# Scores of the dense stage's RWKV units on 64 by 64 quarters of TensorE, without the masked quarter

## The reference

```python
# r, k, v: 4 x 8 x 768 x 48 (batch, heads, tokens, head width); w, u: 8 x 48
for t in range(S):
    cur = einsum('bhd,bhe->bhde', u * k[t], v[t])
    y[:, :, t] = einsum('bhd,bhde->bhe', r[t], state + cur)
    state = w * state + einsum('bhd,bhe->bhde', k[t], v[t])
x = y as 3072 x 384
x = (silu(x @ w_gate) * (x @ w_val)) @ w_out           # dense, 384 -> 1536 -> 384
out = gate * sigmoid * (relu(x @ w1[e]) @ w2[e])        # e: the expert of the row's largest logit
```

## Time and profile before

| what | value |
|---|---|
| median of 3 runs | 874.12 us (874.0 to 876.14) |
| the profiled execution, its own time | 870.95 us |
| its span, first to last instruction | 869.0 us |
| TensorE busy | 844.3 us, 97% |
| VectorE busy | 537.6 us, 62% |
| ScalarE busy | 314.9 us, 36% |
| GpSimd busy | 175.3 us, 20% |
| granted TensorE clock, mean | 0.992 |

### The profile page before, as it was taken

How to read it: one execution, slowest core, us unless ns; L and a number is a source line. 1 busy time by engine, 2 the same in 40 slices (tenths; PEclk the granted TensorE clock), 3 DMA queues, 4 the chain that set the end, 5 groups by cost and what they waited for, 6 DMA issues and landing times. The chain is left out here.

```text
span 869.0 us, 16447 instructions
## 1 busy us (share of the span) xinstructions
PE 844.3 (97%) x6107; PEld 739.0 (85%) x6107; DVE 537.6 (62%) x1063; ACT 314.9 (36%) x500; POOL 175.3 (20%) x141
## 2 busy tenths in 40 slices
PE   7699999999999999999999999999999999999995
PEld 6578888788878888878788878899899999999995
DVE  8667746564566445544444446469969777887770
ACT  1223223111311131112211221347457666687651
POOL 3543302242133403240101001003121101111010
PEclk9799999999999999999999999999999999999999
DMA  9764420352024302340011002537986668766700
GB/s 362 269 210 135 149 92 12 88 172 66 0 65 137 131 1 66 103 133 1 10 46 38 1 2 63 230 137 255 376 325 246 238 245 321 261 247 249 274 17 19
DMA packets 37282, 125.78 MB, mean 145 GB/s; under 512 B 4236, under 2 KB 21056, under 8 KB 31600
## 3 DMA queue, kind: packets, MB, share of 16 engines
q1 hardware_dynamic: 32848, 108.14, 35.3%
q0 software_dynamic: 3520, 9.87, 3.0%
q10 hardware_dynamic: 864, 7.08, 2.2%
HBM read 107.26 MB, written 18.88 MB: 145 GB/s over the span
## 5 line engine op out<-in xcount | busy, mean ns | idle before, releaser
L1607 PE MATMUL bank<-X1H,WH 128*128 128x512 f32 x432 | 169.1, 392 | 2.0 <-DVE YS L1008 1.7
L1607 PE MATMUL bank<-X1L,WH 128*128 128x512 f32 x432 | 168.2, 389 | 0.0
L1607 PE MATMUL bank<-X1H,WL 128*128 128x512 f32 x432 | 168.2, 389 | 0.0
L1243 DVE TENSOR_TENSOR TT<-bank,SG 128x512 f32<-128x512 f32 x72 | 49.7, 691 | 137.5 <-ACT SG L807 137.4
L807 ACT ACTIVATE SG<-bank 128x512 f32<-128x512 f32 x72 | 43.0, 598 | 240.0 <-PE bank L1607 240.0
L737 ACT ACTIVATE AH<-PP 128x512 fp32r<-128x512 f32 (+1 forms) x78 | 46.1, 598 | 158.4 <-DVE PP L1248 158.4
L1607 PEld LDWEIGHTS bank<-X1H,WH 128*128 128x128 f32 x432 | 81.1, 188 | 20.5 <-issue 3.4
L1607 PEld LDWEIGHTS bank<-X1H,WL 128*128 128x128 f32 x432 | 81.1, 188 | 17.1
L1607 PEld LDWEIGHTS bank<-X1L,WH 128*128 128x128 f32 x432 | 81.1, 188 | 16.5
L1653 PE MATMUL bank<-AH,WH 128*128 128x512 f32 (+1 forms) x234 | 91.5, 391 | 0.0
L1655 PE MATMUL bank<-AH,WL 128*128 128x512 f32 (+1 forms) x234 | 87.8, 375 | 0.0
(11 more groups left out here) (229 smaller groups left out, 1798.5 us busy)
## 6 DMA issues: line engine op xcount, KB each, us to landing
W_EVEN<-w SPq DMA_DIRECT2D x20, 1536.0 KB, 8.3
W_ODD<-w SPq DMA_DIRECT2D x18, 1536.0 KB, 8.1
RK_IN<-unit_rk SPq DMA_DIRECT2D x18, 736.0 KB, 5.7
V_IN<-unit_v SPq DMA_DIRECT2D x18, 448.0 KB, 3.4
STG<-w_dense ACTq DMA_DIRECT2D x6, 1152.0 KB, 6.5
mixed<-YS SPq DMA_DIRECT2D x40, 96.0 KB, 2.1
X<-mixed SPq DMA_DIRECT2D x5, 768.0 KB, 4.5
XG_ODD<-store SPq DMA_DIRECT2D x9, 394.0 KB, 8.2
```

What stands on the lines that cost most here:

```text
L1243: tt(TT[:, :], GATE_PS[:, :], SG[:, :], ALU.mult).then_inc(gate_free, 1)
L1607: last = mm(bank_[:, :], lhs[:, f, m, k * P:k * P + P], rhs[:, k, :], start=(x == 0), stop=(x == len(terms) - 1))
```

## The change

Two functions change, for the 18 units of the dense stage alone. In `scores` each head's matmul is cut by keys: the first 64 keys (`EARLIER`) against all 128 queries, the last 64 keys (`LATER`) against the last 64 queries. The quarter of late keys and early queries, which the mask makes zero, is no longer computed. Both pieces have 64 weight columns, so each lies on one quarter of the array. In `mask_scores` the product of each bank is cut in the same way, into 64x512 and 64x4x64; the late-key, early-query part of AM is not written by these units. It holds the zeros that the units ahead of the stage wrote there. A `nop` now carries the wait for `y_added`.

```diff
+EARLIER, LATER = slice(0, P // 2), slice(P // 2, P)
...
                 for half in range(2):
                     dve.wait_ge(scores_ready, 2 * u.i + half + 1)
-                    tt(u.am[:, half, :, :], u.scores[half][:, :].rearrange("p (j t) -> p j t", j=PAIRS),
-                       mask.unsqueeze(1).broadcast_to([P, PAIRS, P]), ALU.mult).then_inc(masked, 1)
+                    made = u.scores[half][:, :].rearrange("p (j t) -> p j t", j=PAIRS)
+                    strict = mask.unsqueeze(1).broadcast_to([P, PAIRS, P])
+                    if u.start:
+                        last = tt(u.am[:, half, :, :], made, strict, ALU.mult)
+                    else:
+                        tt(u.am[EARLIER, half, :, :], made[EARLIER, :, :], strict[EARLIER, :, :], ALU.mult)
+                        last = tt(u.am[LATER, half, :, LATER], made[LATER, :, LATER], strict[LATER, :, LATER], ALU.mult)
+                    last.then_inc(masked, 1)
...
                     pe.wait_ge(y_added, u.behind)
+                    pe.nop(nofuse=True)
                 for s in range(PAIRS):
                     for x in range(2):
                         a = Head(HEAD_AT[x][s])
-                        last = mm(u.scores[x][:, a.keys], u.kw[a.rows, a.keys], u.rw[a.rows, a.keys], start=True, stop=True)
+                        r, w = u.rw[a.rows, a.keys], u.kw[a.rows, a.keys]
+                        if u.start:
+                            last = mm(u.scores[x][:, a.keys], w, r, start=True, stop=True)
+                        else:
+                            to = u.scores[x][:, a.keys]
+                            mm(to[EARLIER, :], w[:, EARLIER], r, start=True, stop=True)
+                            last = mm(to[LATER, LATER], w[:, LATER], r[:, LATER], start=True, stop=True)
                         if s == PAIRS - 1:
                             last.then_inc(scores_ready, 1)
```

## The result

| | before | after |
|---|---|---|
| median of 6 runs each, same chip | 874.06 us (872.27 to 876.14) | 868.95 us (867.91 to 870.28) |
| the profiled execution, its own time | 870.95 us | 867.91 us |
| its span | 869.0 us | 866.1 us |
| TensorE busy | 844.3 us | 839.8 us |
| VectorE busy | 537.6 us | 559.6 us |

The ratio is 0.994, with an interval of 0.9924 to 0.9957: faster by more than the 0.3% that can be told. So the change is worth some 3 us, as the two spans say (2.9), and the first comparison was the luckiest of three.

What follows compares the result with a forecast made beforehand. TensorE's own instruction list was taken as the bound; 17 units x 0.21 us = 3.6 us saved, VectorE's added work hidden, so the median goes from 874.1 to 870.5 us, range 869.0 to 874.8.

Steps and rivals of the forecast that it cites:

- The border goes: TensorE between key sums and scores: sharing quarters removes both losses at the shape change, 0.21 us a unit with 0.02 streaming gain.
- 17 units x 0.21 = 3.6 us.: TensorE, dense stage: 17 of the 18 changed units each save 0.21 us, 3.6 us in all.
- The range, 874.0 - 4.1 - 0.9 = 869.0: Low end of forecast time: lowest earlier run, less 18 x 0.23 us best saving, less 0.9 for run spread.
- A late piece costs nothing beside an early one.: TensorE scores: 64-column late pieces, 0.06 us apart, fit two beside two early ones, which keep 0.11 us a group.
- Rival 2: TensorE scores: issue bounds the 32 passes; at 0.034 us each the gain is eaten, 874.1 us, chance 15%.
- Rival 3, the list's order across quarters: TensorE scores: passes start in list order across quarters, +0.27 us a unit, 878.7 us, chance 11%.
- Rival 1, part of the border stays: TensorE ahead of scores: waits or nop hold them until key sums leave; only 1.5 us won, 872.6 us, chance 14%.
- VectorE +0.75 us a unit, hidden.: VectorE mask: two added 256-column products cost 0.75 us a unit, 13 us in all, covered by idle, so no time.
- The first dense unit gives nothing.: TensorE behind the 18th unit's scores waits 1.68 us for own_key, held by a YS store; saving there 0.

Runs made afterwards that it cites:

- e4: e2 with the late keys against all 128 queries, so the masked quarter is computed again; 872.81 us against 875.67 before, ratio 0.9959.
- e8: e2 with each dense unit's first pair of heads on halves of the array again; 879.46 us against 876.53 before, ratio 1.0032.
- e5: e2 with own_key ahead of AL and the row turn behind scores in first steps of blocks 1 to 4; 872.16 us against 876.53 before.
- e6: e2 with every second head pair's keys turned by 64, evening the quarters, and start units on quarters; 874.27 us against 876.53 before.
- e2: Changed kernel with the old mask over whole banks, scores still on quarters; 872.94 us against 875.67 before, ratio 0.9962.
- e3: Kernel before with only the mask cut in pieces, scores as before; 877.19 us against 875.67, ratio 1.0009.
- e12: e5 and e6 combined, plus stores of YS ahead of loads and a late row turn in the expert stage; 865.23 us against 873.97 before.

## Why the prediction was right or wrong

- **"The border goes", 0.09 + 0.10 + 0.02.** Right, in place and size: 0.218 us measured in 13 units, 0.21 forecast. e4 and e8 separate it from the masked quarter: the quarter gone or not, the distance is 1.471; a border more, 1.828. The Trainium skill's rule (TensorEngine Tiling (Array Packing), Key Properties) that a change of tiling mode drains and a change of tile does not agrees with these rows: 0.20 us ahead of scores in another shape, some 0.1 in the same. That neither waits nor nop drain is shown by the starts after (189.19, 0.48 after the key sums); the kernel without the nop was not tried.
- **"17 units x 0.21 = 3.6 us."** This is the step of the mechanism that failed: the number of units. In the four first-step units nothing was saved, and it should have read 13 x 0.21 = 2.7. The prediction looked there at TT alone. But in step 0 no down projection stands between the scores and the next gate, whose first matmul waits for `own_key` to have read the key sums in the same bank. YS comes 0.85 us after the key sums' start and takes 0.74; no wait for it stood in the trace before, and 0.20 us stand there now. The same chain was seen, and priced at nothing, for the first dense unit; it was not looked for in the others. e5 mends it: all 17 units stand at 1.471. This error made the forecast too large, so it is not why the time came out below it: with 13 units the sum is 871.4 us, further from 868.95 than 870.5 is.
- **The range, 874.0 - 4.1 - 0.9 = 869.0.** This is the term that put the time outside. It allowed the best sum and 0.9 us of spread under 874.0, the lowest of three runs of before, and the median of the first comparison came out 0.05 us below. 3 runs say too little of the spread: before's lowest was 872.27 in the first comparison and 870.17 in the last, and the changed kernel's medians in three comparisons lie between 868.95 and 873.24. The first comparison beat the kernel's own gain by some 2 us, which no term foresaw; that its 5.1 us lie above the forecast of 3.6, and not below it as 2.4 and 2.9 do, is the luck of that comparison.
- **"A late piece costs nothing beside an early one."** Right: early pieces keep 0.11 a group with 32 passes in 0.99 us, 0.031 each over the whole (190.18 - 189.19). Rival 2 needed 0.034 each. It is refuted: e4, with 32 full passes, has the same distance, and in e6 32 passes take 0.79 us, 0.025 each.
- **Rival 3, the list's order across quarters.** Refuted. Late pieces that stand last in the list start at 189.76, and early ones still start at 189.96 (a narrow window, below). The Trainium skill's rule (TensorE: Matmul & The Clock Gate, Part 3, The mechanism) that matmuls start and end strictly in program order does not hold here for the starts on quarters with unequal column counts; the measurement decides. Of the ends it says nothing, as they are modelled.
- **Rival 1, part of the border stays.** Refuted: the whole 0.11 goes at the first start.
- **"VectorE +0.75 us a unit, hidden."** The cover held (e2 and e3), the size was off: +1.0 us a unit, against 0.75. In the whole trace the mask's lines are busy for 43.7 us (24.5, 15.4 and 3.8) where they had 26.9, 17 more against 13. The page's 22 hold more than that: AL grew from 53.7 to 59.5 us, WL by 1.9, and the state's product (ST) fell by 3.7. AL grew in e3 too and not in e2, so it comes with the cut mask: four ALs in block 0 take 2.0 us each, where the usual one takes 0.69, and start beside a GpSimd product. Why is open; no term had it. The step took pieces as if they overlap like two products of one shape (0.64 each); a product of 512 followed by one of 256 on 64 partitions takes 0.69 + 0.46, one after the other. 0.14 us of idle were left ahead of TT where 0.26 were forecast, and TT's own slack behind that.
- **The first dense unit gives nothing.** Neither shown nor refuted: the wait for YS behind it is 0.6 to 4.0 us long in the traces, with and without the change, so a share of 0.2 can't be seen.

## What to carry to other kernels

A change of the tile's shape between neighbouring small matmuls can cost as much as the columns that a smaller tile saves (0.22 us a unit against 0.21 here, and those only with the load evened); ask first what each quarter still streams, for the fullest one sets the time, and work taken from another is worth nothing until the load is evened. When a saving is multiplied by the number of places, check in each place what the next instruction waits for: the same unit in the first step of a block has another neighbour and another limit. And where a wait of some microseconds varies from run to run on the busiest engine, look at the granted clock behind it too, and time both kernels again, before comparing medians 3 us apart.

## What the runs showed of the hardware

Passes on quarters start out of the list's order when their lengths differ. The narrow window at 190.16 to 190.17 of the changed kernel shows what is in flight there:

```profile
189.96 0.29 PE L1543 MATMUL bank<-RW,KW 48*64 48x128 f32 x2
```

That is two groups after the last late piece's start (189.76). The last instruction in the list is such a late piece, and `scores_ready` is raised by it. What the trace does not show is the semaphore against the early pieces' ends; if it goes up with its own piece, it comes ahead of the last early passes. In the first step of block 2 these end, by the modelled ends, at 234.44, and the mask starts at 234.48. Whoever builds on this should let the longest piece raise the semaphore, as e12 does: there the two last pieces in the list are the long ones of their quarters.

The price of a pass on a quarter follows its own columns: 0.109 us for 128. In e6 and e12 a quarter with four passes of 128 and four of 64 takes 0.206 us less than one with eight of 128, so an estimate for 64 is 0.058. The granted clock was 1.00 throughout.
